# Attention by head with 64 stationary columns, two chunks of w_in split on VectorE, and the first loads dealt out anew

## The chip, the cores and the metric

The kernel runs on one core of a Trainium2 chip. The metric is the device time of one execution in microseconds (us), median of three runs. The profiled execution is one more execution; its span is counted from its first to its last instruction.

Names: PE is TensorE (matmuls), PEld its weight loads, DVE is VectorE, ACT is ScalarE, POOL is GpSimd, SP is SyncE, which here only issues DMAs. SPq and ACTq are the DMA issues of SP and ACT. "f32" matmuls of the attention come as two records each, and one weight load goes with each record. The products of the first network use the single-pass type fp32r and have one record each.

## The reference

```python
# q, k, v: [4, 8, 576, 64]; causal window of 64 positions
scores = q @ k.T / sqrt(64); masked outside the window; attn = softmax(scores)
x = (attn @ v) as rows [2304, 512]
h = x @ w_in                       # [512, 2048]
x2 = (h - tanh(h)) @ w_out         # [2048, 512]
# eight experts, one for each row, chosen by argmax of a scaled cosine with expert_emb
out[rows of e] = gate * (relu(x2[rows] @ w1[e]) @ w2[e])   # 512 -> 1024 -> 512
```

## The kernel before, in words

The work is split by hand over the engines; each engine runs its own written-out order and waits on semaphores.

**Attention** goes by group g, 48 of them. A group is one pair of heads and three blocks of 64 queries. Its steps: `transpose_qk` (PE), `evacuate` (DVE), `score` (PE), `mask_max` (DVE), `exp` (ACT), `pad_sum` and `invert` (DVE), `normalise` (POOL, line 502), `transpose_p` (PE, line 1156), `copy_pT` (ACT), `attend` (PE, line 1170: p with v), `copy_x` (ACT), `split_x` (POOL, lines 510 and 512: x as a high and a low part). The score matrix of a block has the 128 keys of its window as rows and, as columns, 64 queries of one head beside 64 of the other.

`attend` holds the v of both heads (128 columns) stationary and streams all 128 columns of p, three times for a group. Of each 128x128 result only the two 64x64 blocks on the diagonal are used, one for each head.

**The front.** The first eight groups (`FIRST = 8`) run alone, in a loop over j in which each engine has its pieces of up to five groups. Every matrix of the first network is held as a high and a low fp32r part, and the high-high, high-low and low-high products are summed. w_in comes in five loads and is split in 16 chunks of 128 columns by `split_w_in` (POOL, lines 519 and 521: a cast and a subtraction). The first two chunks are split inside the front's loop, at j = 4 and 5. Chunk c is needed by `first_product(0, c)`.

**The main loop** goes over 6 blocks of 384 rows and 16 chunks c of the hidden dimension: `first_product` (12 matmuls of 128x384), `second_product` (9 of 128x512), and between them pieces of the remaining 40 groups. After it come the routing and the experts, which load, split and use w1 and w2.

**Loads of the front.** Queues are in order. SP issues q and k of the pairs of heads, then v of pairs 2 and 3, then the first part of w_in. ACT issues k of pair 0 and v of pairs 0 and 1, then begins with its first `exp`.

Of the kernel before, what the change touches and what calls it, by code (L numbers as in the profile page):

```python
# [9 lines left out]
ALU = mybir.AluOpType  # L10
# [3 lines left out]
P = 128  # L14
# [20 lines left out]
def build(nc, q, k, v, w_in, w_out, emb, tau, w1, w2, out):  # L35
    B, H, S, D = q.shape
# [4 lines left out]
    NB, PAIRS, GB = S // WINDOW, H // 2, 3  # L41
# [23 lines left out]
    with ExitStack() as ctx:  # L65
        def sb(name, shape, dt=F32, scope=ctx):
            return scope.enter_context(nc.sbuf_tensor(name, shape, dt))

        def sem(name):
            return ctx.enter_context(nc.semaphore(name))  # L70

        def sems(name, n):
            return [sem(f"{name}{i}") for i in range(n)]
# [46 lines left out]
        vw = [sb(f"vw{i}", [P, 2 * GB, 2, D], scope=attn) for i in range(2)]  # L120
# [4 lines left out]
        pT = [sb(f"pT{i}", [P, GB, P], scope=attn) for i in range(2)]  # L125
# [10 lines left out]
        win_h = sb("win_h", [P, KC, F], F32R, phase1)  # L136
        loading = ExitStack()
        win_raw = sb("win_raw", [P, KC, F], scope=loading)
        loading.close()
        win_l = sb("win_l", [P, KC, F], F32R, phase1)  # L140
# [64 lines left out]
        ident_made, masks_made, pads_zeroed, consts_made = sem("ident_made"), sem("masks_made"), sem("pads_zeroed"), sem("consts_made")  # L205
        small_loaded, en_scaled, en_transposed, en_ready = sem("small_loaded"), sem("en_scaled"), sem("en_transposed"), sem("en_ready")
        table_cleared = sem("table_cleared")
        first_qk_loaded, first_v_loaded = sems("first_qk_loaded", PAIRS + 1), sems("first_v_loaded", PAIRS)
        qk_loaded, v_loaded = sems("qk_loaded", 2), sems("v_loaded", 2)
        win_loaded, win_high, win_split = sems("win_loaded", 5), sem("win_high"), sem("win_split")  # L210
        qk_transposed, qk_evacuated = sem("qk_transposed"), sem("qk_evacuated")
        carried = sem("carried")
# [29 lines left out]
        def grouped(bank):  # L242
            return banks[:, bank, 0:GB * P].rearrange("p (g c) -> p g c", g=GB)
# [6 lines left out]
        def psS(g):  # L250
            return grouped((1, 2)[g % 2] if g < FIRST else 5)
# [4 lines left out]
        def psO(g):  # L256
            return grouped((7, 4)[g % 2] if g < FIRST else 6)
# [23 lines left out]
        def window_of(g):  # L281
            return 2 * (g // FIRST) + g % 2
# [6 lines left out]
        def buffer_of(u):  # L289
            return u if u < PAIRS else u % 2  # L290

        def parts(u):
            one, two = 2 * (u // PAIRS), 2 * (u // PAIRS) + 1
            if one // GP == two // GP:
                return ((one, 0, 2 * GB),)
            return (one, 0, GB), (two, GB, 2 * GB)
# [55 lines left out]
        def load_blocks(eng, blocks, to, u, part, loaded):  # L352
            w, start, end = part
            for h in range(2):
                at = (H * (w // GP) + 2 * (u % PAIRS) + h) * NB + GB * (w % GP)
                eng.dma_start(to[:, start:end, h, :], blocks[:, at:at + end - start, :]).then_inc(loaded, 16)

        def load_q(eng, u, part, loaded):
            load_blocks(eng, q_blocks, qk[buffer_of(u)][0:WINDOW], u, part, loaded)

        def load_k(eng, u, part, loaded):
            load_blocks(eng, k_blocks, qk[buffer_of(u)][WINDOW:P], u, part, loaded)
# [3 lines left out]
        def load_v(eng, u, loaded):  # L366
            hp, to = u % PAIRS, vw[buffer_of(u)]
            for w, start, end in parts(u):
                at = (H * (w // GP) + 2 * hp) * S + GT * (w % GP)
                skip = 1 if w % GP == 0 else 0  # L370
                if skip:
                    eng.dma_start(to[WINDOW:P, start, :, :], v[w // GP, 2 * hp:2 * hp + 2, 0:WINDOW, :].rearrange("h p d -> p h d")).then_inc(loaded, 16)
                for h in range(2):
                    overlapping = bass.AP(v.tensor, (at + h * S + WINDOW * (skip - 1)) * D, [[D, P], [WINDOW * D, end - start - skip], [1, D]])
                    eng.dma_start(to[:, start + skip:end, h, :], overlapping).then_inc(loaded, 16)
# [4 lines left out]
        def _(sp):  # L380
# [22 lines left out]
            load_q(sp, 0, (1, GB, 2 * GB), first_qk_loaded[0])  # L403
            for u in range(1, PAIRS):
                load_q(sp, u, parts(u)[0], first_qk_loaded[u])
                load_k(sp, u, parts(u)[0], first_qk_loaded[u])
            sp.wait_ge(pads_zeroed, 2)
            load_v(sp, 2, first_v_loaded[2])
            load_v(sp, 3, first_v_loaded[3])
            load_win(0)  # L410
            load_qk_unit(PAIRS)
            load_wout(0)
# [63 lines left out]
        def _(pool):  # L476
# [37 lines left out]
            def split_w_in(c):  # L514

                cols = slice(c * P, (c + 1) * P)
                i = next(i for i in range(5) if WIN_COLS[i + 1] > c * P)
                pool.wait_ge(win_loaded[i], 16)
                pool.tensor_copy(win_h[:, :, cols], win_raw[:, :, cols]).then_inc(win_high, 1)
                pool.wait_ge(win_high, c + 1)  # L520
                pool.tensor_tensor(win_l[:, :, cols], win_raw[:, :, cols], win_h[:, :, cols], ALU.subtract).then_inc(win_split, 1)

            def constants(part):
# [34 lines left out]
            for j in range(FIRST + 5):  # L558
                if 3 <= j < FIRST + 3:
                    normalise(j - 3)  # L560
                if j in (4, 5):
                    split_w_in(j - 4)
                if 5 <= j:
                    split_x(j - 5)

# [67 lines left out]
        def _(act):  # L633
# [26 lines left out]

            load_k(act, 0, (0, 0, GB), first_qk_loaded[PAIRS])
            load_k(act, 0, (1, GB, 2 * GB), first_qk_loaded[0])
            act.wait_ge(pads_zeroed, 2)
            for u in range(2):
                load_v(act, u, first_v_loaded[u])
            for j in range(FIRST + 5):
                if 1 <= j < FIRST + 1:
                    exp(j - 1)
# [147 lines left out]
        def _(dve):  # L816
# [25 lines left out]
            def mask_max(g, units):  # L842

                for u in units:
                    last = dve.tensor_tensor_reduce(sm[g % 4][:, u, :], psS(g)[:, u, :], (mask0 if window_of(g) % GP == 0 and u == 0 else mask)[:],
                                                    -1.0, -2.0 * MASKED, ALU.add, ALU.min, nmx[:, g % 4, u:u + 1])
                if units[-1] == GB - 1:
                    last.then_inc(maxed, 1)
# [9 lines left out]
            for j in range(FIRST + 3):  # L858
                if j < FIRST:
                    evacuate(j)  # L860
                if j == 1:
                    dve.wait_ge(masks_made, 1)
                masks, inverts = 1 <= j <= FIRST, 3 <= j
                if masks:
                    dve.wait_ge(scored, j)
                    wait(dve, p_transposed, j - 4)
                if inverts:
                    pad_sum(j - 3)
                if masks:
                    mask_max(j - 1, [0])  # L870
                if inverts:
                    invert(j - 3)
                if masks:
                    mask_max(j - 1, [1, 2])

            def pieces(s):
                if (g := begun(s, 0)) is not None:
# [241 lines left out]
        def _(pe):  # L1119
# [39 lines left out]
            def attend(g):  # L1159
                u, a = g // 2, g % 2  # L1160
                pe.wait_ge(pT_copied, g + 1)
                if g < FIRST:
                    wait(pe, x_copied, g - 1)

                if a == 0 and g < FIRST:
                    pe.wait_ge(first_v_loaded[u], 16 * loads_of_v(u))
                elif a == 0:
                    pe.wait_ge(v_loaded[u % 2], 16 * sum(loads_of_v(before) for before in earlier(u)))
                for v in range(GB):
                    last = pe.matmul(psO(g)[:, v, :], vw[buffer_of(u)][:, GB * a + v, :, :].rearrange("p h d -> p (h d)"), pT[g % 2][:, v, :],  # L1170
                                     start=True, stop=True)
                last.then_inc(attended, 1)

            for j in range(FIRST + 5):
# [26 lines left out]
            def first_product(n, c):  # L1201
                u = FC * n + c
                if c == 0:
                    pe.wait_ge(x_split, FIRST * n + FIRST)
                if n == 0:
                    pe.wait_ge(win_split, c + 1)

                wait(pe, g_ready, u - 1)
                cols = slice(c * P, (c + 1) * P)
                for kk in range(KC):  # L1210
                    last = products(psH[c % 2], (win_h[:, kk, cols], win_l[:, kk, cols]),
                                    [x[:, kk, n % 2, :, :].rearrange("p w t -> p (w t)") for x in (xh, xl)], kk == 0, kk == KC - 1)
                last.then_inc(h_ready, 1)
# [77 lines left out]
            for st in range(ST):  # L1291
                for kk in range(KC):
                    last = pe.transpose(psX_last[st][:, kk * P:(kk + 1) * P], x2[:, st, kk * P:(kk + 1) * P], ident[:])
                last.then_inc(x2_transposed, 1)
            for st in range(ST):
                pe.wait_ge(x2T_copied, 2 * ST * (NBLK - 1) + st + 1)
                for kk in range(KC):
                    last = pe.matmul(psL[:, st, :], x2T_last[st][:, kk * P:(kk + 1) * P], enT[:, kk, :], start=(kk == 0), stop=(kk == KC - 1))
# [137 lines left out]
```

## Time and profile before

| what | value |
|---|---|
| median of 3 runs | 885.0 us (882.24 to 886.79) |
| profiled execution | 886.58 us |
| its span | 884.8 us |
| PE busy | 828.3 us, 94% |
| PE weight loads busy | 725.1 us, 82% |
| DVE / ACT / POOL busy | 45% / 41% / 23% |

Busy time is the sum of the stretches in which an engine has an instruction under way. PE's records overlap one another, so the distance between the starts of two records tells what one costs, and not its length. The profiled execution is 1.6 us above the median, and its span is 1.8 us below its own time.

### The profile page before, as it was taken

The page shows a single profiled execution, that of the slowest core. Times are in us where ns is not written, and L with a number is a line of the kernel's source. Part 1 is how long each engine was busy: PE and PEld are TensorE (multiplying, and loading weights), DVE is VectorE, ACT ScalarE, POOL GpSimd, SP SyncE. Part 2 cuts the span into 40 slices and gives each one's busy share as a digit, 9 for nine tenths or more (in the row PEclk, how much of TensorE's full clock was granted, in tenths as well). Part 3 has the DMA queues.
Part 4 walks back from the last instruction along what each step waited for, and adds up shares of the span by engine and source line. Part 5 has one row for each costly group of instructions (what it writes and reads, how often), then busy time and mean ns, then how long its engine had stood idle before and what let it go on. Part 6 is the DMA issues. An engine that isn't in the chain of part 4 may idle for free. (4 is left out here: it accounts for less than half of the span.)

```text
span 884.8 us, 15973 instructions
## 1 busy us (share of the span) xinstructions
PE 828.3 (94%) x4496; PEld 725.1 (82%) x4497; DVE 397.8 (45%) x1207; ACT 362.8 (41%) x880; POOL 201.7 (23%) x288
## 2 busy tenths in 40 slices
PE   5689999999999999999999999569999999999992
PEld 4579998898899889988899999547888888888872
DVE  6146654454445444544553333555526161455412
ACT  4435554334433443344333222515625263555423
POOL 2737641112111211121112001121111111111111
PEclk9789999999999999999999999889999999999995
DMA  9951222111211121112003400016643341655110
GB/s 174 260 177 36 57 50 72 37 35 35 71 35 35 36 58 48 37 37 72 20 1 72 155 1 1 36 38 225 220 144 124 109 160 47 231 214 216 60 39 22
DMA packets 100531, 77.33 MB, mean 87 GB/s; under 512 B 78364, under 2 KB 79521, under 8 KB 100466
## 3 DMA queue, kind: packets, MB, share of 16 engines
q1 hardware_dynamic: 92098, 64.28, 24.5%
q0 software_dynamic: 4624, 11.32, 4.1%
q10 hardware_dynamic: 3744, 0.92, 0.6%
q8 instruction: 34, 0.56, 0.3%
q14 instruction: 31, 0.25, 0.1%
HBM read 142.39 MB, written 11.44 MB: 174 GB/s over the span
## 5 line engine op out<-in xcount | busy, mean ns | idle before, releaser
L1197 PE MATMUL banks<-xh,win_h 128*128 128x384 f32 x384 | 137.1, 357 | 2.1 <-POOL xl L512 2.1
L1199 PE MATMUL banks<-xh,win_l 128*128 128x384 f32 x384 | 130.7, 340 | 0.0
L1198 PE MATMUL banks<-xl,win_h 128*128 128x384 f32 x384 | 130.1, 339 | 0.0
L905 DVE TENSOR_TENSOR gf<-banks,gf 128x384 f32<-128x384 f32 x96 | 53.5, 557 | 153.9 <-ACT gf L687 153.9
L687 ACT ACTIVATE gf<-banks 128x384 f32<-128x384 f32 x96 | 47.2, 492 | 183.9 <-PE banks L1199 183.9
L1197 PE MATMUL banks<-wout_h,gh 128*128 128x512 f32 x288 | 119.2, 414 | 0.0
L1199 PE MATMUL banks<-wout_h,gl 128*128 128x512 f32 x288 | 113.6, 394 | 0.0
L1198 PE MATMUL banks<-wout_l,gh 128*128 128x512 f32 x288 | 112.7, 391 | 0.0
L502 POOL TENSOR_TENSOR sm<-sm,rr 128x384 f32<-128x384 f32 x48 | 42.0, 874 | 298.6 <-DVE rr L856 298.6
L909 DVE TENSOR_TENSOR gl<-gf,gh 128x384 fp32r<-128x384 f32 x96 | 55.1, 574 | 112.4 <-ACT gh L694 107.7
L694 ACT CAST gh<-gf 128x384 fp32r<-128x384 f32 x96 | 49.2, 512 | 128.4 <-PE banks L1199 127.2
L1197 PEld LDWEIGHTS banks<-xh,win_h 128*128 128x128 f32 x384 | 73.1, 190 | 2.9 <-POOL xl L512 2.3
L1198 PEld LDWEIGHTS banks<-xl,win_h 128*128 128x128 f32 x384 | 73.3, 191 | 0.6
L1090 DVE TENSOR_TENSOR hTl<-banks,hTh 128x512 fp32r<-128x512 f32 x50 | 32.3, 687 | 92.0 <-ACT hTh L780 91.5
L1197 PE MATMUL banks<-w1h,xgh 128*128 x176 | 70.8, 402 | 2.8 <-DVE xgl L1098 1.7
L1199 PEld LDWEIGHTS banks<-xh,win_l 128*128 128x128 f32 x384 | 72.9, 190 | 0.0
L1197 PE MATMUL banks<-w2h,hTh 128*128 x176 | 70.8, 402 | 0.9 <-DVE hTl L1090 0.9
L1199 PE MATMUL banks<-w1h,xgl 128*128 x176 | 68.9, 392 | 0.0
L1199 PE MATMUL banks<-w2h,hTl 128*128 x176 | 68.9, 391 | 0.0
L1198 PE MATMUL banks<-w2l,hTh 128*128 x176 | 68.6, 390 | 0.0
L1198 PE MATMUL banks<-w1l,xgh 128*128 x176 | 68.5, 389 | 0.0
L1199 PEld LDWEIGHTS banks<-wout_h,gl 128*128 128x128 f32 x288 | 54.0, 188 | 12.5
(185 smaller groups left out, 1485.9 us busy)
## 6 DMA issues: line engine op xcount, KB each, us to landing
w1raw<-in_moe_w_dram SPq DMA_DIRECT2D x104, 512.0 KB
w2raw<-in_moe_w_dram SPq DMA_DIRECT2D x104, 512.0 KB
x_rows<-x SPq DMA_DIRECT2D x6, 768.0 KB, 3.8
wout_raw<-in_moe_w_out_dram SPq DMA_DIRECT2D x4, 1024.0 KB, 6.9
win_raw<-in_moe_w_in_dram SPq DMA_DIRECT2D x3, 1024.0 KB, 10.0
vw<-in_v_dram SPq DMA_DIRECT2D x16, 192.0 KB, 3.0
qk<-in_q_dram SPq DMA_DIRECT2D x30, 96.0 KB, 2.6
qk<-in_k_dram SPq DMA_DIRECT2D x30, 96.0 KB, 2.7
```

What stands on the lines that cost most here:

```text
L502: pool.tensor_tensor(sm[g % 4][:], sm[g % 4][:], rr[:, g % 4, :].unsqueeze(2).broadcast_to((P, GB, P)), ALU.mult).then_inc(normed, 1)
L687: act.activation(gf[c % 2][:], psH[c % 2], ACT.Tanh).then_inc(tanh_ready, 1)
L694: act.copy(gh[c % 2][:], gf[c % 2][:]).then_inc(g_high, 1)
L905: dve.tensor_tensor(gf[c % 2][:], psH[c % 2], gf[c % 2][:], ALU.subtract).then_inc(g_ready, 1)
L909: dve.tensor_tensor(gl[c % 2][:], gf[c % 2][:], gh[c % 2][:], ALU.subtract).then_inc(g_split, 1)
L1090: dve.tensor_tensor(hTl[:, part, :], psHT[half].rearrange("p (k t) -> p k t", k=KC), hTh[:, part, :], ALU.subtract).then_inc(hT_split, 1)
L1197: pe.matmul(to, sh, mh, start=start, stop=False)
L1198: pe.matmul(to, sh, ml, start=False, stop=False)
L1199: return pe.matmul(to, sl, mh, start=False, stop=stop)
```

## The change

Three things are done. `attend` works by head: two matmuls with 64 stationary and 64 moving columns in place of each one with 128 and 128; each writes its own 64 partitions of the result. DVE splits chunks 0 and 1 of w_in, behind all its work of the front, with two semaphores of their own; POOL keeps chunks 2 to 15. SP issues all q of the front and then all v, ACT all k.

```diff
             load_q(sp, 0, (1, GB, 2 * GB), first_qk_loaded[0])
             for u in range(1, PAIRS):
                 load_q(sp, u, parts(u)[0], first_qk_loaded[u])
-                load_k(sp, u, parts(u)[0], first_qk_loaded[u])
             sp.wait_ge(pads_zeroed, 2)
-            load_v(sp, 2, first_v_loaded[2])
-            load_v(sp, 3, first_v_loaded[3])
+            for u in range(PAIRS):
+                load_v(sp, u, first_v_loaded[u])
             load_win(0)
...
-                pool.wait_ge(win_high, c + 1)
+                pool.wait_ge(win_high, c - 1)
...
-                if j in (4, 5):
-                    split_w_in(j - 4)
...
             load_k(act, 0, (1, GB, 2 * GB), first_qk_loaded[0])
-            act.wait_ge(pads_zeroed, 2)
-            for u in range(2):
-                load_v(act, u, first_v_loaded[u])
+            for u in range(1, PAIRS):
+                load_k(act, u, parts(u)[0], first_qk_loaded[u])
...
+            dve.wait_ge(win_loaded[0], 16)
+            for c in range(2):
+                cols = slice(c * P, (c + 1) * P)
+                dve.tensor_copy(win_h[:, :, cols], win_raw[:, :, cols]).then_inc(first_win_high, 1)
+                dve.wait_ge(first_win_high, c + 1)
+                dve.tensor_tensor(win_l[:, :, cols], win_raw[:, :, cols], win_h[:, :, cols], ALU.subtract).then_inc(first_win_split, 1)
...
                 for v in range(GB):
-                    last = pe.matmul(psO(g)[:, v, :], vw[buffer_of(u)][:, GB * a + v, :, :].rearrange("p h d -> p (h d)"), pT[g % 2][:, v, :],
-                                     start=True, stop=True)
+                    for h in range(2):
+                        own = slice(h * D, (h + 1) * D)
+                        last = pe.matmul(psO(g)[own, v, own], vw[buffer_of(u)][:, GB * a + v, h, :], pT[g % 2][:, v, own],
+                                         start=True, stop=True)
...
-                if n == 0:
-                    pe.wait_ge(win_split, c + 1)
+                if n == 0 and c < 2:
+                    pe.wait_ge(first_win_split, c + 1)
+                elif n == 0:
+                    pe.wait_ge(win_split, c - 1)
```

POOL's order in the front, before. L502 is `normalise`, L519 and L521 are `split_w_in`, L510 and L512 are `split_x`:

```order
L502 TENSOR_TENSOR sm<-sm,rr 128x384 x2
L519 CAST win_h<-win_raw 128x4x128
L521 TENSOR_TENSOR win_l<-win_raw,win_h 128x4x128
L502 TENSOR_TENSOR sm<-sm,rr 128x384
L519 CAST win_h<-win_raw 128x4x128
L521 TENSOR_TENSOR win_l<-win_raw,win_h 128x4x128
L510 CAST xh<-xraw 128x192
L512 TENSOR_TENSOR xl<-xraw,xh 128x192
```

And now:

```order
L502 TENSOR_TENSOR sm<-sm,rr 128x384 x3
L510 CAST xh<-xraw 128x192
L512 TENSOR_TENSOR xl<-xraw,xh 128x192
L502 TENSOR_TENSOR sm<-sm,rr 128x384
L510 CAST xh<-xraw 128x192
```

The third `normalise` no longer stands behind a wait for w_in.

PE's order at the end of the front, now (line 1177 is `attend` in the changed file, lines 1204 to 1206 the products):

```order
L1161 MATMUL banks<-ident,sm 128x128 x3
L1177 MATMUL banks<-pT,vw 64x64 x6
L1161 MATMUL banks<-ident,sm 128x128 x3
L1177 MATMUL banks<-pT,vw 64x64 x12
L1204 MATMUL banks<-xh,win_h 128x384
L1205 MATMUL banks<-xl,win_h 128x384
```

Before, the same place had (line 1170 is `attend`):

```order
L1156 MATMUL banks<-ident,sm 128x128 x3
L1170 MATMUL banks<-pT,vw 128x128 x3
L1156 MATMUL banks<-ident,sm 128x128 x3
L1170 MATMUL banks<-pT,vw 128x128 x6
L1197 MATMUL banks<-xh,win_h 128x384
L1198 MATMUL banks<-xl,win_h 128x384
```

Each group's three matmuls became six of a quarter of the size; nothing moved around them, here and in the main loop.

## Rows read from the trace of the kernel before

**Rows 1.** Windows by stage: us, busy us of each engine (records), PE clock, DMA share, GB/s.

```profile
0.00:44.00 44.00, 26.27 (x145) 23.24 (x146) 17.98 (x103) 19.72 (x74) 22.41 (x52) 0.88 0.93 216
44.00:60.00 16.00, 12.88 (x58) 11.98 (x59) 7.31 (x27) 4.57 (x13) 4.89 (x6) 0.79 0.70 243
60.00:480.00 420.00, 419.95 (x2465) 378.24 (x2464) 206.12 (x768) 173.81 (x532) 114.23 (x173) 1.00 0.18 41
```

**Rows 2.** Timeline of PE in the front: start us, length us, work [idle before <-releaser].

```profile
10.44 0.90 PE L1136 MATMUL banks<-ident,qk 128*128 128x128 f32 x3 [2.21 <-DMA qk<-in_k_dram]
...
24.91 0.90 PE L1156 MATMUL banks<-ident,sm 128*128 128x128 f32 x3 [3.91 <-POOL sm L502]
...
30.73 0.87 PE L1145 MATMUL banks<-kT,qbd 128*128 128x128 f32 x6
31.43 0.49 PE L1156 MATMUL banks<-ident,sm 128*128 128x128 f32 x3
...
43.92 0.44 PE L1197 MATMUL banks<-xh,win_h 128*128 128x384 f32 x1 [2.09 <-POOL xl L512]
```

**Rows 3.** Timeline of POOL in the front.

```profile
22.12 0.61 POOL L519 CAST win_h<-win_raw 128x512 fp32r<-128x512 f32 x1 [4.25 <-DMA win_raw<-in_moe_w_in_dram]
22.81 1.26 POOL L521 TENSOR_TENSOR win_l<-win_raw,win_h 128x512 fp32r<-128x512 f32 x1
24.03 0.83 POOL L502 TENSOR_TENSOR sm<-sm,rr 128x384 f32<-128x384 f32 x1
24.80 0.61 POOL L519 CAST win_h<-win_raw 128x512 fp32r<-128x512 f32 x1
...
26.70 0.34 POOL L510 CAST xh<-xraw 128x192 fp32r<-128x192 f32 x1
```

**Rows 4.** Windows of 5 us around that wait.

```profile
20.00:25.00 5.00, 1.09 (x11) 0.90 (x9) 1.83 (x11) 2.81 (x13) 2.80 (x4) 0.90 0.53 133
25.00:30.00 5.00, 5.00 (x24) 5.00 (x25) 1.62 (x6) 1.11 (x3) 4.22 (x7) 0.50 1.13 325
```

**Rows 5.** Timeline of the DMA issues of SP and ACT.

```profile
3.81 0.62 ACTq L372 DMA_DIRECT2D vw<-in_v_dram  x1
...
4.83 1.29 SPq L356 DMA_DIRECT2D qk<-in_k_dram  x2
...
15.91 0.70 SPq L393 DMA_DIRECT2D win_raw<-in_moe_w_in_dram  x1
```

**Rows 6.** Timeline of DVE: its last work of the front, and later `low_w_out`.

```profile
34.91 0.17 DVE L856 RECIPROCAL rr<-rse 128x3 f32<-128x3 f32 x1
48.27 0.56 DVE L905 TENSOR_TENSOR gf<-banks,gf 128x384 f32<-128x384 f32 x1 [13.18 <-ACT gf L687]
...
51.72 0.69 DVE L901 TENSOR_TENSOR wout_l<-wout_raw,wout_h 128x512 fp32r<-128x512 f32 x1
```

**Rows 7.** Timeline of PE around one `attend` of the main loop.

```profile
143.01 0.83 PE L1170 MATMUL banks<-pT,vw 128*128 128x128 f32 x6
143.60 0.42 PE L1197 MATMUL banks<-xh,win_h 128*128 128x384 f32 x1
143.85 0.34 PE L1198 MATMUL banks<-xl,win_h 128*128 128x384 f32 x1
144.03 0.35 PE L1199 MATMUL banks<-xh,win_l 128*128 128x384 f32 x1
```

**Rows 8.** `attend` in the main loop, all of it: durations in ns, first and last start.

```profile
L1170 PE MATMUL banks<-pT,vw x240: 270/275/275, 66.0 to 476.4; 128*128 128x128 f32 x120
```

**Rows 9.** Timeline of PE around `logits`: 128 stationary, 8 moving columns.

```profile
165.35 0.96 PE L1253 MATMUL banks<-enT,x2T 128*128 128x8 f32 x8
166.16 0.42 PE L1245 MATMUL banks<-ident,x 128*128 128x128 f32 x2
```

**Rows 10.** Timelines of PE and PEld around `transpose_emb`: stationary of 8 rows.

```profile
94.09 0.40 PE L1199 MATMUL banks<-wout_h,gl 128*128 128x512 f32 x1
94.42 0.41 PE L1232 MATMUL banks<-ident,embn 8*128 8x8 f32 x4
94.76 0.44 PE L1197 MATMUL banks<-xh,win_h 128*128 128x384 f32 x1
95.04 0.34 PE L1198 MATMUL banks<-xl,win_h 128*128 128x384 f32 x1
...
94.42 0.32 PEld L1232 LDWEIGHTS banks<-ident,embn 8*128 8x128 f32 x4 [0.36 <-issue]
94.76 0.19 PEld L1197 LDWEIGHTS banks<-xh,win_h 128*128 128x128 f32 x1
```

More of the change, by code:

```diff
@@ L209, in build @@
         qk_loaded, v_loaded = sems("qk_loaded", 2), sems("v_loaded", 2)
+        first_win_high, first_win_split = sem("first_win_high"), sem("first_win_split")
         win_loaded, win_high, win_split = sems("win_loaded", 5), sem("win_high"), sem("win_split")
```

## The prediction, written before the changed kernel ran

> **What bounds the kernel now.** I read the windows by stage first [rows 1]. In 60 to 480 us PE has no idle time (419.95 of 420.00 us) at a granted clock of 1.00, while DVE, ACT and POOL are busy for half of it or less. So there the time is PE's own: what a piece of attention adds to PE is added to the kernel. In the first 44 us no engine is full: PE is busy 26.27 us and POOL 22.41. That is a chain from engine to engine, and what counts is which wait ends last. Whatever the front gains carries through, since the main loop behind it waits for nothing but PE.
>
> In the front the timeline of PE [rows 2] has three waits that the change touches: 2.21 us at 10.44 for k of pair 1; 3.91 us at 24.91 for POOL's `normalise` of group 2; and at 43.92 the first product, released by the last `split_x`. POOL's timeline tells why `normalise` was late [rows 3]: POOL stood 4.25 us in front of `split_w_in(0)` until the load of w_in landed at 22.12, split until 24.03, and only then normalised. After it comes the second split, 24.80 to 26.70. The stall costs once more: the granted clock is 0.50 (the 1.2 GHz level) in 25 to 30 us, where PE is full, after a stretch with 1.09 us of PE work in 5 [rows 4].
>
> **The front, part by part.** *Splits off POOL.* This takes 4.25 us of waiting and two splits of about 1.9 us each from between POOL's pieces. What PE had of it is 3.91 us. The second split of 1.90 us is felt only in part, since PE was full from 24.91 to past 31.43 [rows 2]. But that stretch ran at half clock: scores take 0.70 us there from start to start once the clock is back (30.73 to 31.43), and twice that before.
>
> *Splits on DVE.* DVE gets two casts and two subtractions of 512 columns behind its last `invert`. A subtraction of this size took 0.69 us [rows 6]; a cast lies between nothing and the same. So 1.4 to 2.8 us, and I take 2.4. DVE's last `invert` was at 34.91, its next work at 48.27 [rows 6], so 13 us lay free. The queue behind the new wait (the first `less_tanh`) needs the first product anyway. Even if `invert` comes at 28 us, w_in has landed (22.12) and the splits end by 31, before the first product. Cost: nothing. Without that cover it would be 2.4 us once.
>
> *Loads.* Both queues issue as many DMAs as before: on SP six loads of k leave and six of v come, on ACT six of v leave and six of k come. So w_in is still issued near 15.9 us [rows 5] and ACT begins its first `exp` as before. k of pair 1 moves from 4.83 on SP to 3.81 on ACT [rows 5], and six loads of v no longer run ahead of the later q and k. I expect the 2.21 us wait to shrink by some 1.9. v of pair 0 comes at about 8 us, long before the first `attend`.
>
> Sum of the front: the bound below is 3.91 (only POOL's stall goes), above is 3.91 + 2.21 + 1.90 + about 2 for a better clock = 10. I followed the loop piece by piece, each engine in its order, with the durations of the rows. This gives the first product at 43.9 before and at about 37 after, **a gain of 7 us**, of which 2 hang on the loads.
>
> **`attend`, part by part.** Before: PE starts it at 143.01 and the second product record behind it at 143.85 [rows 7]. One 128x384 record takes 0.18 us (143.85 to 144.03), so the group costs 0.84 - 0.18 = 0.67 us, six records of 0.11. Is that the stream or the weight load? `logits` has 8 records with 8 moving columns, and they take 166.16 - 165.35 = 0.81 us, 0.10 each [rows 9]. An f32 record with 128 stationary columns thus costs about 0.11 however few columns stream: **the weight load bounds it**. 120 matmuls of this kind (240 records, 40 groups) lie in the full stretch [rows 8].
>
> After: 12 records a group. No row has f32 loads of fewer columns. The bounds: if a load is as long as before, 0.11 each and 12 x 0.11 = 1.34 us; if it goes with its columns, 0.056 to 0.06 and 0.70 us. The nearest row is that of `transpose_emb`, whose four loads start 0.06 apart ((0.32 - 0.14) / 3) [rows 10], so steps of 0.06 are possible. I take 0.06, that is 0.72.
>
> The second term: PE changes the part of the array that it uses. `transpose_emb` is the one place in this trace that does (8 rows in place of 128). Its load is not pulled ahead of the product before it: 0.36 us idle with nothing waited for, and the load behind it starts late too [rows 10]. From 94.09 to 95.04 are 0.95 us; less 0.23 for the 512-column record and 0.17 for the 384-column one, 0.54 remain for four records, of which 4 x 0.06 = 0.24 are their own. **Leaving the full array and coming back cost 0.30 us.** For `attend` I take the same 0.30 for each group; below it could be nothing, if columns are another case than rows, above 0.5, if the longer loads and streams are waited out too.
>
> So 0.72 + 0.30 = 1.02 against 0.67: +0.35 a group, x 40 = **+14 us**. The eight groups of the front are on the chain in part (the last two wholly): +0.35 x 4 = +1.5.
>
> The Trainium skill, "TensorEngine Tiling", section Key Properties, says that changing the tiling mode, not just the tile, drains the engine; the gap in rows 10 agrees with it, and by it each group pays twice, going and coming back. The skill, "TensorE: Matmul & The Clock Gate", section LDWEIGHTS, gives load time by columns, which would put the halved loads at the lower bound.
>
> **Sum.** -7 + 14 + 1.5 = +8.5. On the profiled execution's 886.6 this is 895; on the median of 885.0 it is **893.5 us**. What lies behind 60 us only moves later or earlier; loads of w1 and w2 wait for the last `attend`, which moves with the rest.
>
> **Rivals.**
> 1. *No price for the narrower part (ends not slower).* If a 64-column load is pulled ahead like any other, a group costs 0.72, +0.05 x 40 = +2, and with the front's -7 the time is 880. Against it: rows 10. For it: those are 8 rows and a transpose, not 64 columns. It decides from the switch price: below about 0.12 us the front's gain outweighs it. Chance 0.20.
> 2. *The two heads run side by side.* Each uses its own 64 columns. Then a group is six steps of 0.06 = 0.36, plus 0.30: 0.66, no change, and the front leaves 878; with no switch price 0.36, -12, and 866. No row shows two streams at once. Chance 0.12. The same page, "TensorEngine Tiling", Key Properties, says that different tiles can load and multiply in parallel.
> 3. *Loads don't shrink, or load and stream of a head take turns.* 0.11 a record: 1.34 a group, +27, and with the switch price +39. Less 7 for the front: 905 to 917. Chance 0.12.
> 4. *The front gains nothing, the price is paid.* If w_in's landing or the chain of DVE and ACT takes the place of POOL's stall: 885 + 15.5 = 900. DMA is full at 325 GB/s in 25 to 30 us [rows 4], so a new wait for w_in's later parts is thinkable. Chance 0.06.
>
> The forecast itself has 0.50, with a range of its own of 886 to 901 (switch price 0.15 to 0.45, front 4 to 10).
>
> **How the numbers follow.** A measurement of this kernel tells about 0.5% (4.4 us) from no change. Faster by more (below 880.6): rival 2 and half of rival 1, 0.22. Within: half of rival 1 and the forecast's lower edge, 0.17. Slower: 0.61. The range reaches over rivals 1 and 4 and the nearer half of rival 2: 874 to 906. It leaves out the far ends of rivals 2 and 3.
>
> **What would show it.** In the changed trace: the first product near 37 us in place of 43.9; no POOL wait for w_in in the front; DVE's splits done before the first product. In the main loop: whether PE's 64x64 loads start before the product ahead of them has streamed, how far their records are apart (0.06 or 0.11), and how long it takes from the first record of `attend` to the second product record behind it (0.84 before, 1.2 by the forecast, 0.9 by rival 1). The prediction is wrong if that distance is not between 1.0 and 1.4, or if the clock in the main loop falls below 1.00 because PE now pauses 40 times.

## The result: 0.6% faster, where 1% slower was forecast

The changed kernel takes 879.45 us (median of 5 runs, 878.8 to 881.48) against 885.91 us. The ratio is 0.9939, with a 95% interval of 0.9915 to 0.9963: 5.4 us less (3.3 to 7.5). One of the 29 executions of the kernel before that stand beside experiments 1 to 4 took 2626 us and is left out of their ratios. The forecast was 893.5 us, with a range of 874 to 906 that holds the measured time, but the forecast had the wrong sign.

The windows by stage of the changed kernel (us, busy us of each engine with its records, PE clock, DMA share, GB/s) answer to [rows 1]:

```profile
0.00:37.00 37.00, 23.23 (x193) 18.56 (x195) 21.69 (x107) 19.62 (x74) 20.07 (x48) 0.90 0.90 198
37.00:44.00 7.00, 4.93 (x22) 4.65 (x22) 2.19 (x6) 1.52 (x3) 3.25 (x4) 0.74 1.10 355
44.00:60.00 16.00, 14.69 (x87) 13.19 (x87) 9.16 (x32) 6.82 (x23) 5.80 (x6) 0.92 0.72 234
60.00:480.00 420.00, 419.93 (x2690) 366.03 (x2690) 203.92 (x758) 169.36 (x523) 109.57 (x169) 1.00 0.19 45
```

The main loop is as full as before and at full clock. What moved is the front. Its timeline of PE, with the places of [rows 2]:

```profile
8.15 0.90 PE L1141 MATMUL banks<-ident,qk 128*128 128x128 f32 x3
...
18.84 0.49 PE L1161 MATMUL banks<-ident,sm 128*128 128x128 f32 x3
...
21.69 0.55 PE L1161 MATMUL banks<-ident,sm 128*128 128x128 f32 x3 [0.69 <-POOL sm L502]
...
36.63 0.69 PE L1204 MATMUL banks<-xh,win_h 128*128 128x384 f32 x1 [2.13 <-POOL xl L512]
...
42.76 1.42 PE L1150 MATMUL banks<-kT,qbd 128*128 128x128 f32 x6 [2.07 <-DVE kT L837]
```

The transpose that stood 2.21 us for k now starts at 8.15 without a wait. `transpose_p` of group 2, which stood 3.91 us for `normalise` and started at 24.91, starts at 18.84 without a wait; the line at 21.69 is group 3, and the longest wait of that kind left is 1.79 us. And the first product starts at 36.63 in place of 43.92. POOL and DVE, their timelines, answer to [rows 3] and [rows 6]:

```profile
17.25 0.83 POOL L502 TENSOR_TENSOR sm<-sm,rr 128x384 f32<-128x384 f32 x1 [1.17 <-DVE rr L853]
19.84 0.34 POOL L510 CAST xh<-xraw 128x192 fp32r<-128x192 f32 x1 [1.76 <-ACT xraw L651]
```

```profile
27.19 0.40 DVE L877 CAST win_h<-win_raw 128x512 fp32r<-128x512 f32 x1
27.62 0.84 DVE L879 TENSOR_TENSOR win_l<-win_raw,win_h 128x512 fp32r<-128x512 f32 x1
28.38 0.81 DVE L877 CAST win_h<-win_raw 128x512 fp32r<-128x512 f32 x1
29.22 1.20 DVE L879 TENSOR_TENSOR win_l<-win_raw,win_h 128x512 fp32r<-128x512 f32 x1
40.91 0.56 DVE L910 TENSOR_TENSOR gf<-banks,gf 128x384 f32<-128x384 f32 x1 [10.49 <-ACT gf L684]
```

Group 2 is normalised at 17.25 in place of 24.03. DVE's four pieces end at 30.42 (29.22 + 1.20), six us ahead of the first product, in time that it would have idled.

Now the place where the forecast saw 14 us. Timelines of PE and of PEld around one `attend` of the main loop, answering to [rows 7], and the line over the whole execution:

```profile
135.57 0.39 PE L1205 MATMUL banks<-wout_l,gh 128*128 128x512 f32 x1
135.80 0.39 PE L1206 MATMUL banks<-wout_h,gl 128*128 128x512 f32 x1
136.12 0.57 PE L1177 MATMUL banks<-pT,vw 128*64 128x64 f32 x12
136.62 0.45 PE L1204 MATMUL banks<-xh,win_h 128*128 128x384 f32 x1
136.90 0.34 PE L1205 MATMUL banks<-xl,win_h 128*128 128x384 f32 x1
...
136.12 0.43 PEld L1177 LDWEIGHTS banks<-pT,vw 128*64 128x64 f32 x12 [0.35 <-ACT pT L642]
136.62 0.19 PEld L1204 LDWEIGHTS banks<-xh,win_h 128*128 128x128 f32 x1
```

```profile
L1177 PE MATMUL banks<-pT,vw x576: 222/222/369, 17.3 to 469.9; 128*64 128x64 f32 x192
```

Twelve records span 0.57 us, the last of them 0.22 long: twelve starts lie within 0.35 us. At 0.06 each, one after another, they would need 0.66. From 136.12 to 136.90 are 0.78 us, less than the 0.84 of before. What is new is ahead of the group: from 135.80 to its first record it takes 0.32 us where a 512-column product takes 0.23 (135.57 to 135.80). So a group costs 0.78 + 0.09 - 0.18 = 0.69 us, against 0.67 before and 1.02 in the forecast. The profile puts the 0.35 us in which PEld is idle down to ACT's `copy_pT`, which had ended at 135.83. It is not that wait: in eight of the groups `copy_pT` had ended 1.39 us or more before, and the profile names no releaser ("issue"), yet the four of them that stand behind a 512-column product start 0.33 us behind it, as the others do. So I read the gap as part of the change of the array:

```profile
PEld banks L1177 <- ACT pT L642: 11.0, 31, 0.4
PEld banks L1177 <- issue: 2.5, 8, 0.4
```

### The profile page after: what moved, and what is told of

It reads as the page before. It is cut to its first block and busy times, and to the rows that moved or that the text cites. A ratio compares the mean times of both kernels' runs of the same rounds, so it can differ in the third digit from the quotient of the medians.

```text
span 878.1 us, 16549 instructions
## 1 busy us (share of the span) xinstructions
PE 825.0 (94%) x4784; PEld 707.2 (81%) x4785; DVE 401.8 (46%) x1211; ACT 360.9 (41%) x880; POOL 198.9 (23%) x284
## 5 line engine op out<-in xcount | busy, mean ns | idle before, releaser
L502 POOL TENSOR_TENSOR sm<-sm,rr 128x384 f32<-128x384 f32 x48 | 42.1, 876 | 298.2 <-DVE rr L853 298.2
```

Of the source, the lines that this page charges most:

```text
L502: pool.tensor_tensor(sm[g % 4][:], sm[g % 4][:], rr[:, g % 4, :].unsqueeze(2).broadcast_to((P, GB, P)), ALU.mult).then_inc(normed, 1)
```

## The experiments

The runs below were made on three chips; each is compared with the kernel before on its own chip, and runs of different chips by their ratios.

**Theory A**: the two heads of a block use different columns of the array and run side by side, so that 12 records cost six steps of 0.058 us; going to the narrow part and back costs about 0.34 us a group; the two nearly cancel, and all of the gain is the front's. Rivals: the gain is `attend`'s (B), or a small record is simply four times cheaper in any order.

**1. attend by head alone**, in the kernel before:

```diff
-  last = pe.matmul(psO(g)[:, v, :], vw[...], pT[g % 2][:, v, :], ...)
+  for h in range(2):
+      last = pe.matmul(psO(g)[own, v, own], vw[...][:, ..., h, :], pT[g % 2][:, v, own], ...)
```

> The kernel before, with attend by head as the only edit; splits and loads as before. Theory A (the two heads' matmuls run side by side, six steps of 0.058 us, plus about 0.34 us for going to the narrow part and back): a group costs 0.69 us in place of 0.67, so 40 groups add 1.0 us; in the front a full-array attend at half clock took 1.28 us and this one less, which may give back up to 1 us there. Expected 885 to 887, no change. Theory B (the gain of the changed kernel comes from attend, not from the front): 879 to 881.

Measured: 885.52 us against 883.83 of before on the same chip, ratio 1.0019 (1.0005 to 1.0034): slower by 0.4 to 3.0 us, 1.7 in the middle. Theory B falls; A's 1.0 us lies inside. The mean granted clock of these twelve runs is 0.968, that of the kernel before beside them 0.973; how much of the 1.7 us is `attend`'s own work is read in run 8.

**2. The front alone** (the changed kernel, its `attend` put back):

> The changed kernel with attend as before (128 stationary columns): splits on DVE and the new loads alone. Theory A: it keeps the front's gain of about 7.3 us and has not the 1.0 us that 40 groups of attend by head lose, so about 878.5, first product at 36.6 to 37.2 us. Theory B: near 885.

Measured: 878.98 us, ratio 0.9942 (0.9924 to 0.9959), 5.1 us less than before, with the first product at 36.40. The front makes the whole gain. That it beats the changed kernel by 1 us is neither shown nor excluded: the two ratios differ by 0.0003, and their intervals are ten times as wide. The profiles can tell it (run 8).

**3. The splits alone**, loads and `attend` as before:

```diff
-                if j in (4, 5):
-                    split_w_in(j - 4)          # POOL
+            dve.wait_ge(win_loaded[0], 16)     # DVE, behind its front
+            (chunks 0 and 1: tensor_copy, tensor_tensor)
```

> The kernel before, with only the two chunks of w_in split on DVE; loads and attend as before. If my split of the front's gain holds, POOL's stall and the second split give about 5 of the 7 us: about 881, first product near 39 us, and the 2.2 us wait for k at 10.4 us still there. Rival: the stall only moves to the next wait of the chain and the loads carry the gain: 884 to 886.

Measured: 881.54 us, ratio 0.9979 (0.9968 to 0.9989): 1.9 us less (1.0 to 2.8), where the expectation gave this part about 5 of the 7 us. Its profile has the first product at 39.18 and the wait for k still there. PE's timeline:

```profile
10.27 0.90 PE L1143 MATMUL banks<-ident,qk 128*128 128x128 f32 x3 [2.08 <-DMA qk<-in_k_dram]
...
39.18 0.44 PE L1204 MATMUL banks<-xh,win_h 128*128 128x384 f32 x1 [2.09 <-POOL xl L513]
```

The profile says -4.7 us at the first product and the timed runs say -1.9 at the end. Run 8 takes this up.

**4. The loads alone**:

```diff
-  SP: q0, q1 k1, q2 k2, q3 k3, v2, v3        ACT: k0, v0, v1
+  SP: q0, q1, q2, q3, v0, v1, v2, v3         ACT: k0, k1, k2, k3
```

> The kernel before, with only the loads dealt out anew (SP all q then all v, ACT all k). The first groups come about 2 us earlier, but POOL still stands in front of w_in until about 22 us, so that nearly all of it is lost again: 885 to 886, first product near 43.9 us. If the two edits simply add up: 883.5 to 884.

Measured: 884.48 us, ratio 1.0004 (0.999 to 1.0018): nothing that the timed runs can show. PE's timeline:

```profile
8.54 0.90 PE L1134 MATMUL banks<-ident,qk 128*128 128x128 f32 x3 [0.34 <-DMA qk<-in_k_dram]
...
23.64 0.90 PE L1154 MATMUL banks<-ident,sm 128*128 128x128 f32 x3 [4.76 <-POOL sm L501]
```

The first groups come 1.9 us sooner and then stand longer, 4.76 us in place of 3.91, before the same POOL that waits for w_in. w_in itself landed sooner too (20.85 in place of 22.12), so that 1.3 us are left behind this wait (23.64 in place of 24.91). The first product starts at 41.68, not near 43.9 as expected; why nothing of this reaches the end is taken up in run 8. Alone, the splits give 1.9 us and the loads nothing; together 5.1. Each edit uncovers the other.

**5. One head after the other**, in the changed kernel:

```diff
-                for v in range(GB):
-                    for h in range(2):
+                for h in range(2):
+                    for v in range(GB):
```

> The changed kernel, with the two loops of attend exchanged: the three matmuls of head 0, then the three of head 1, so that neighbours use the same 64 columns. Work, shapes and number of changes to the narrow part are the same. Theory A (neighbours overlap only because they use different columns): 12 steps of 0.058 us in place of six, +0.35 us a group, +14 us: about 893, with the records 0.058 apart one by one. Rival (a record with 64 stationary and 64 moving columns simply costs 0.029 us, a quarter, in whatever order): 879.5, no change against the changed kernel.

Measured: 885.52 us against 884.21, ratio 1.0017 (1.0002 to 1.0032). That is 0.78% or 6.9 us over the changed kernel: the order matters, so a small record is not cheap by itself. But it is half of the 14 us. Timelines of PE and PEld:

```profile
136.61 0.73 PE L1177 MATMUL banks<-pT,vw 128*64 128x64 f32 x12
137.28 0.44 PE L1204 MATMUL banks<-xh,win_h 128*128 128x384 f32 x1
137.56 0.34 PE L1205 MATMUL banks<-xl,win_h 128*128 128x384 f32 x1
...
136.61 0.59 PEld L1177 LDWEIGHTS banks<-pT,vw 128*64 128x64 f32 x12 [0.35 <-ACT pT L642]
```

The twelve starts now lie within 0.73 - 0.22 = 0.51 us, between the 0.35 of the pairs and the 0.64 of eleven steps of 0.058. A group takes 0.95 us in place of 0.78: +0.17, times 40 is 6.8 us, which is what the runs show. The records one by one show why. The twelve starts, in us after the first, are two rows of six with the same steps, 0.11 once and then 0.058: 0, 0.11, 0.16, 0.22, 0.28, 0.34, and 0.17, 0.28, 0.34, 0.39, 0.45, 0.51 (all 39 groups in 60 to 480 us). In the changed kernel they are 0, 0.11, 0.16, 0.22, 0.28, 0.34 for both heads, 0.007 us apart. So the second head starts 0.17 us after the first, when three of the first head's six records had yet to start: PE took records of the second head ahead of those of the first that were still waiting. That is why theory A's 14 us came only by half.

**6. Twice to the narrow part in each group**: the middle block of `attend` with the full array.

```diff
+                    if v == 1:
+                        pe.matmul(psO(g)[:, v, :], vw[...both heads...], pT[g % 2][:, v, :], ...)
+                        continue
```

> The changed kernel, but the middle of the three matmuls of a group is done with the full array (128 stationary columns), the first and third by head: each group goes to the narrow part and back twice in place of once. Theory A with the price at each round trip (0.34 us): 4 steps of 0.058 + 2 of 0.112 + 2 x 0.34 = 1.14 us a group against 0.69, +18 us: about 897. If the price is paid once for a group only: 0.80, +4 us: about 884. If there is none: 0.46, and about 870.

Measured: 898.94 us, ratio 1.0173 (1.0145 to 1.0201), 2.3% or 21 us over the changed kernel. PE's timeline:

```profile
141.72 0.34 PE L1181 MATMUL banks<-pT,vw 128*64 128x64 f32 x4
141.98 0.49 PE L1176 MATMUL banks<-pT,vw 128*128 128x128 f32 x2
142.40 0.34 PE L1181 MATMUL banks<-pT,vw 128*64 128x64 f32 x4
142.67 0.44 PE L1208 MATMUL banks<-xh,win_h 128*128 128x384 f32 x1
142.95 0.34 PE L1209 MATMUL banks<-xl,win_h 128*128 128x384 f32 x1
```

A group takes 142.95 - 141.72 = 1.23 us, +0.45, and 40 x 0.45 = 18 us (most of the rest lies ahead, in the front, where the other eight groups are): the price is paid at each round trip. A round trip more, 2 steps of 0.058 less and 2 of 0.112 more come to price + 0.11, so the price is 0.34 us.

**7. `evacuate` ahead of `less_tanh`** on DVE, in the kernel of experiment 2. The profile of the changed kernel had shown PE's loads waiting 11.0 us in 31 waits for DVE in 60 to 480 us, a wait that neither kernel addresses:

```diff
+                    if (g := begun(s, 0)) is not None:
+                        evacuate(g)
                     less_tanh(n, c)
-                    pieces(s)      # began with evacuate(g)
+                    pieces(s)      # without it, for the same s
```

> The front of the changed kernel with attend as before, and in the main loop DVE does evacuate ahead of less_tanh instead of behind it. In the changed kernel's profile PE's loads wait for evacuate (kT) 31 times in 60 to 480 us, 11.0 us in all, and 3.4 us in two waits in 40 to 52 us. If those waits are PE's own time, most of 4 to 9 us goes: 870 to 875. If PE's matmuls in flight cover them, or the late less_tanh costs as much: 877 to 879.

Measured: 871.71 us, ratio 0.9863 (0.9836 to 0.989): 12 us less than before, 7 less than experiment 2 by the two ratios, the fastest of all. The waits of 60 to 480 us (us in total, times, longest), first of experiment 2, then of this:

```profile
PEld banks L1150 <- DVE kT L837: 11.0, 30, 0.4
```

```profile
DVE qbd L831 <- PE banks L1143: 54.1, 31, 2.6
```

In the second no wait of PE or PEld for DVE is left; DVE waits for PE instead, and DVE has the time. The kernel before has the same wait (10.9 us in 30 waits). The matmuls tell it too. In experiment 2 the score of a group is preceded by a gap (130.12 to 130.50, where a 512-column record takes 0.23):

```profile
130.12 0.39 PE L1204 MATMUL banks<-wout_h,gl 128*128 128x512 f32 x1
130.50 0.94 PE L1150 MATMUL banks<-kT,qbd 128*128 128x128 f32 x6
131.19 0.42 PE L1202 MATMUL banks<-xh,win_h 128*128 128x384 f32 x1
```

```profile
127.84 0.39 PE L1206 MATMUL banks<-wout_h,gl 128*128 128x512 f32 x1
128.07 0.83 PE L1152 MATMUL banks<-kT,qbd 128*128 128x128 f32 x6
128.66 0.42 PE L1204 MATMUL banks<-xh,win_h 128*128 128x384 f32 x1
```

1.07 us from the record ahead to the one behind become 0.82: 0.25 us for each of some 30 groups, 7.5 us, in a stretch whose window says that PE was busy for 419.92 of 420.00 us.

**8. Second profiles**: the kernel before twice more, the splits alone and the changed kernel once more.

> The kernel before once more, unchanged, for a second profile. The one of before shows the first product at 43.92 us and a clock of 0.79 in 44 to 60 us; with the splits on DVE alone the profile shows 39.18 us and yet only 1.9 us less time by the timed runs. If the half-clock stretches fall differently in each execution, this profile has the first product somewhere in 41.5 to 44 us and a span that differs from 884.8 by 1 to 3 us. If the front is the same each time: 43.9 and 884.8 within 0.3 us.

> A third profile of the kernel before, same question: where the half-clock stretches fall, and when the first and the third chunk's products start.

> A second profile of the kernel with the splits on DVE alone. If its first product is again at 39.2 within 0.3 us while the two new profiles of before scatter, the front of before is what varies from execution to execution.

> A second profile of the changed kernel. First product again at 36.6 us within 1 us; the distance from the first record of attend to the second product record behind it again 0.78 us, since nothing there depends on the front.

The windows of the first 60 us, in this order: before, its second and third profile, the splits alone twice, the changed kernel twice. The figure before the last two is PE's clock:

```profile
0.00:60.00 60.00, 39.16 (x202) 35.22 (x204) 25.29 (x130) 24.30 (x87) 27.30 (x57) 0.86 0.87 223
```

```profile
0.00:60.00 60.00, 38.33 (x227) 34.07 (x229) 26.82 (x133) 27.05 (x97) 31.05 (x60) 0.97 0.88 226
```

```profile
0.00:60.00 60.00, 38.88 (x208) 34.14 (x210) 25.50 (x131) 24.17 (x87) 28.47 (x58) 0.91 0.88 225
```

```profile
0.00:60.00 60.00, 42.76 (x228) 38.25 (x230) 30.01 (x138) 27.02 (x97) 28.39 (x56) 0.89 0.89 226
```

```profile
0.00:60.00 60.00, 41.56 (x232) 37.27 (x234) 30.98 (x140) 27.01 (x97) 28.35 (x56) 0.91 0.89 226
```

```profile
0.00:60.00 60.00, 42.85 (x299) 36.40 (x301) 33.04 (x145) 27.97 (x100) 29.12 (x57) 0.89 0.88 226
```

```profile
0.00:60.00 60.00, 42.95 (x297) 36.38 (x299) 32.78 (x145) 27.68 (x99) 28.81 (x57) 0.86 0.87 226
```

The kernel before had its first product at 43.92, 42.51 and 42.44 us, and spans of 884.8, 881.0 and 884.4. The execution with the clock at 0.97 is the shortest. The one that I predicted from, at 0.86, had the worst clock and the latest first product of the three, so comparing one profile with one profile overstated every gain of the front: the splits alone start their first product at 39.18 and 39.78, which is 2.7 to 4.7 us sooner than before, depending on which two profiles are taken (39.78 is outside the 0.3 us that I had expected). The changed kernel has it at 36.63 and 36.62, 5.8 to 7.3 us sooner, with a clock no better (0.89, 0.86). In both of its profiles a group of `attend` takes 0.78 us in the main loop.

The first product is not the end of the front's scatter. ACT's `tanh` of each chunk is a later mark; here it is from the fifth of block 0 to the last of block 5, with first and last start, for the kernel before three times, experiment 2, and the changed kernel twice:

```profile
L687 ACT ACTIVATE gf<-banks x91: 491/492/495, 74.5 to 554.4; 128x384 f32<-128x384 f32 x91
```

```profile
L687 ACT ACTIVATE gf<-banks x91: 491/492/495, 70.2 to 549.9; 128x384 f32<-128x384 f32 x91
```

```profile
L687 ACT ACTIVATE gf<-banks x91: 490/492/494, 73.2 to 553.2; 128x384 f32<-128x384 f32 x91
```

```profile
L684 ACT ACTIVATE gf<-banks x91: 490/492/494, 67.2 to 547.2; 128x384 f32<-128x384 f32 x91
```

```profile
L684 ACT ACTIVATE gf<-banks x91: 491/492/493, 67.3 to 548.1; 128x384 f32<-128x384 f32 x91
```

```profile
L684 ACT ACTIVATE gf<-banks x91: 490/491/493, 67.6 to 548.2; 128x384 f32<-128x384 f32 x91
```

Two things can be read there. First, the kernel before reaches its fifth `tanh` anywhere from 70.2 to 74.5 us, so its executions differ by 4.3 us ahead of this mark and by 0.9 us at most behind it (810.3, 810.8 and 811.2 us to the end). The loads alone reach it at 72.5, inside that scatter, which fits the missing gain of experiment 4; the splits alone at 70.0 and 69.0. Second, the stretch behind the mark takes 479.6 to 480.0 us in all seven profiles with `attend` and the main loop as before (experiments 2, 3 and 4 among them) and 480.5 to 480.8 in the three with `attend` by head (experiment 1 and the changed kernel twice). So `attend` by head does cost the changed kernel some 0.8 us in the main loop, as 40 x (0.69 - 0.67) says. The same stretch takes 486.8 us in experiment 5 (+6.0), 498.2 in experiment 6 (+17.4) and 473.9 in experiment 7 (6.1 less than in experiment 2; the rest of its 7 us lies ahead of the mark, at 64.8, and may be the clock's, 0.94 in its first 60 us).

## Why the prediction was wrong

**Where it held.** What the front gains carries through: behind the fifth `tanh` the changed kernel takes as long as the kernel before, but for the 0.8 us of `attend`. That the main loop "waits for nothing but PE" did not hold: the kernel before has 10.9 us of waits of PE's weight loads for DVE there, under a PE busy for 419.95 of 420 us, and experiment 7 got some 7 us by removing them. It did no harm to the sum, since the wait is the same before and after (11.0 us). The front came as laid out: first product at 36.6 (37 forecast), POOL without a wait for w_in, DVE's splits (3.23 us from first start to last end, 2.4 forecast) under cover. On the timed runs it is worth 5.1 us (3.6 to 6.7), not 7. Against the profile that it was made from, the first product did come 7.3 us sooner; but that profile, with a clock of 0.86 in its first 60 us, had the latest first product of three. The upper bound also added 2 us for a better clock; it did not get better. The range of "switch price 0.15 to 0.45, front 4 to 10" was also added up too narrowly: by its own terms it runs from 884 to 903, not from 886 to 901.

The part of the loads (2 us) held only in company: nothing alone, about 3 us once the splits are off POOL (5.1 less 1.9, each known to 1 or 1.5 us).

**The price of the narrow part** held as well: 0.30 us was read from a transposition with 8 rows, in one place of the trace [rows 10], and `attend` pays 0.34 (experiment 6). The load going with its columns held too: 0.058 us a step within one head, by experiment 5's records.

**The step that failed** is the one before it: "I take 0.06, that is 0.72", for 12 records in a row. It set twelve steps one behind the other. With neighbours in different columns they are six steps, 0.35 us, and the group costs 0.35 + 0.34 = 0.69 in place of the forecast 1.02. So +14 us became +1, and the front's gain stood alone: -5.1 + 1 = -4.1, against a measured -5.4 (-3.3 to -7.5). The term of +1.5 for the eight groups of the front is not seen in the runs. At half clock a group of `attend` took 1.28 us before (six records of 0.21, at 25.61), and in the changed kernel, at 30.76, it is through in under 1 us: its twelve starts lie within 0.60.

This was rival 2, worked out as 0.36 + 0.30 = 0.66 and 878 us, with 0.12. "No row shows two streams at once" was true and was taken as evidence against it. It was none: the kernel before never used two column halves of the array one behind the other, so no row of its trace could have shown it. The Trainium skill, "TensorEngine Tiling", section Key Properties, says that different tiles can load and multiply in parallel; the order experiment and the twelve starts in 0.35 us agree. I had used that section's line on draining for the forecast and set the line beside it aside.

**Rival 1** (no price) and rivals 3 and 4 fall: experiment 6 shows the price, the records show the halved loads, experiment 2 the front's gain. Rival 1's 880 is near the measured time by accident, since its two errors cancel.

**What stays open.** Whether `attend` by head also costs something outside the main loop: alone it costs 0.4 to 3.0 us in the timed runs, at a granted clock lower than that of the kernel before (0.968 against 0.973), and no run shows why the clock differs. And how much the splits alone are worth: their two profiles start the first product 2.7 to 4.7 us sooner and reach the fifth `tanh` 0.2 to 5.5 us sooner, the timed runs give 1.0 to 2.8. The scatter of the kernel before ahead of that mark is wide enough for it (28 of its runs beside them lie between 881.6 and 886.4 us); a cause beyond it was not looked for.

## What to carry to other kernels

Two small f32 matmuls in the two column halves of the array, side by side, take the time of one, and each trip to the narrow part and back costs a third of a microsecond. By the numbers here a block saves 2 x (0.112 - 0.058) = 0.11 us, so three blocks just pay for one trip (an estimate from these two steps). It pays only where more such pairs stand together and alternate between the halves. When no row of a trace can show an overlap because the program never offered one, that is no evidence against it: work out what it would be worth and keep its chance as it was without that trace. And a window in which PE is busy for 419.92 of 420 us can hide 7 us of waits: read the waits of the weight loads and the distances between starts there.

## What the runs showed of the hardware

- Two f32 matmuls with 64 stationary and 64 moving columns in different halves of the array, over the same 128 rows, run side by side: twelve starts in 0.35 us, in pairs 0.007 us apart. Those of the same half start 0.058 us apart. With all of one half first in program order, those of the other half still started 0.17 us after them, ahead of three that were waiting (0.51 us for the twelve, experiment 5).
- Going from the full array to half of its columns and back costs 0.34 us at full clock, each time (experiment 6).
- An f32 record with 64 stationary and 64 moving columns takes half of the step of one with 128 and 128 (0.058 against 0.112 us), its weight load included.
- The stretches at half clock in the first 60 us fall differently in each execution of one kernel (mean clock 0.86, 0.97 and 0.91); its spans were 884.8, 881.0 and 884.4 us, and the differences arose ahead of 75 us.
